# Bucket mask of an attention kernel built from per-bit rows on VectorE instead of two one-hot products on TensorE

## The reference

```
q_bits = (q @ proj > 0);  k_bits = (k @ proj > 0)        # 6 bits per row
q_bucket = sum(q_bits * 2**n);  k_bucket = sum(k_bits * 2**n)
mask = q_bucket[:, None] == k_bucket[None, :]
scores = where(mask, scale * q @ k.T, -1e9)
attn = exp(scores - max(scores));  attn = attn / (sum(attn) + 1e-9)
out = attn @ v                                            # (2, 8, 768, 64)
```

## Time and profile before

| what | value |
|---|---|
| median of three runs | 616.67 us |
| profiled execution | 616.41 us, of which the span of the trace is 614.7 us |
| attention stage in the trace | first `scores` at 13.15 us, last transposes of pair 8 near 242 us |
| TensorE busy | 605.4 us, 98% of the span |
| VectorE, ScalarE, GpSimd busy | 431.1, 347.6, 349.3 us |
| granted TensorE clock | 9 (90% or more) in all 40 slices |

### The profile page before, as it was taken

The page is one execution under the profiler, slowest core; times in us unless marked ns, Lnnn a source line. Parts: engine busy times, 40 slices in busy tenths (PEclk is TensorE's granted clock), DMA queues, the critical chain, the costliest instruction groups (busy, mean ns, idle before and its releaser), DMA issues.

```text
span 614.7 us, 10917 instructions
## 1 busy us (share of the span) xinstructions
PE 605.4 (98%) x3676; PEld 503.5 (82%) x3676; DVE 431.1 (70%) x689; ACT 347.6 (57%) x700; POOL 349.3 (57%) x337
## 2 busy tenths in 40 slices
PE   7899999999999999999999999999999999999998
PEld 3667777776776776999888999999999999988887
DVE  3988888888888885788676666545677666579920
ACT  3877777777777785354444444335444444264232
POOL 4533434333337756146458988873999999234140
PEclk9999999999999999999999999999999999999999
DMA  6842323233232210001212122113222221100202
GB/s 137 244 118 64 91 66 91 64 90 90 64 90 79 62 46 3 1 2 53 69 51 69 56 64 61 60 57 99 69 85 85 86 86 51 35 1 0 86 19 102
DMA packets 27650, 42.20 MB, mean 69 GB/s; under 512 B 3425, under 2 KB 15713, under 8 KB 27617
## 3 DMA queue, kind: packets, MB, share of 16 engines
q1 hardware_dynamic: 25648, 37.38, 20.9%
q0 software_dynamic: 1728, 4.02, 2.6%
q10 hardware_dynamic: 240, 0.39, 0.3%
HBM read 38.63 MB, written 3.15 MB: 68 GB/s over the span
## 4 chain that ended last, share of the span: by engine, by line
PE 95%; DVE 2%; DMA 1%; ACT 1%; POOL 1%; issue 0%; ACTq 0%; POOLq 0%
PE banks L1882 22%; PE banks L1914 16%; PE banks L1667 12%; PE banks L1684 11%; PE banks L1734 10%; PE banks L1996 5%; PE banks L2012 5%; PE banks L1873 4%; PE banks L1707 2%; PE banks L1818 2%; PE banks L1620 2%; DMA k_raw<-in_k 1%; PE banks L1742 1%; PE banks L1858 1%; PE banks L1626 1%; PE banks L1792 1%
## 5 line engine op out<-in xcount | busy, mean ns | idle before, releaser
L1246 DVE TENSOR_REDUCE row_min<-banks 128x1 f32<-128x768 f32 x96 | 91.8, 956 | 31.8 <-PE banks L1667 31.1
L873 ACT ACTIVATE prob<-banks,row_min 128x768 f32<-128x768 f32 x96 | 87.1, 907 | 29.0 <-DVE row_min L1246 28.9
L1506 DVE TENSOR_TENSOR partial_sums<-banks,partial_sums 128x384 f32<-128x384 f32 x78 | 43.4, 557 | 54.9 <-PE banks L1914 54.7
L1734 PE MATMUL banks<-ident,prob 128*128 128x128 f32 x576 | 79.2, 273 | 1.4 <-ACT probT L374 1.4
L1734 PEld LDWEIGHTS banks<-ident,prob 128*128 128x128 f32 x576 | 68.1, 140 | 6.7 <-issue 1.9
L606 POOL TENSOR_TENSOR k_b<-k_raw,k_a 64x768 fp32r<-64x768 f32 x16 | 29.3, 1829 | 70.7 <-ACT k_a L856 70.7
L1684 PE MATMUL banks<-probT,v_in 128*64 128x384 f32 x384 | 69.0, 494 | 0.0
L1882 PE MATMUL banks<-h_hi,w_hi 128*128 128x512 f32 (+1 forms) x256 | 66.1, 339 | 0.0
L1882 PE MATMUL banks<-h_hi,w_lo 128*128 128x512 f32 (+1 forms) x256 | 65.6, 337 | 0.0
L1882 PE MATMUL banks<-h_lo,w_hi 128*128 128x512 f32 (+1 forms) x256 | 65.3, 336 | 0.0
L374 ACT COPY probT<-banks 128x384 f32<-128x384 f32 x104 | 49.1, 480 | 22.4 <-PE banks L1734 22.1
(11 more groups left out here) (216 smaller groups left out, 1515.0 us busy)
## 6 DMA issues: line engine op xcount, KB each, us to landing
w_stage<-in_moe_w_ch SPq DMA_DIRECT2D x38, 256.0 KB, 2.6
q_raw<-in_q SPq DMA_DIRECT2D x32, 192.0 KB, 3.3
k_raw<-in_k SPq DMA_DIRECT2D x30, 192.0 KB, 3.6
w_pair<-in_moe_w_ch SPq DMA_DIRECT2D x7, 512.0 KB, 3.7
v_in<-in_v SPq DMA_DIRECT2D x16, 192.0 KB, 2.8
w_stage<-in_moe_w_ch SPq DMA_DIRECT2D x6, 512.0 KB, 3.8
out<-y_out SPq DMA_DIRECT2D x11, 256.0 KB, 2.0
seq_tables_sb<-in_dft POOLq DMA_DIRECT2D x6, 386.0 KB, 3.7
```

The costliest lines, as they stand in the source:

```text
L873: act.activation(prob[s % 2][:, :, :], s_tile(s), ACT.Exp, bias=row_min[:, s:s + 1], scale=-1.0, accum_out=row_sum[:, s:s + 1]).then_inc(e ...
L1246: dve.tensor_reduce(row_min[:, s:s + 1], s_tile(s), AX.XY, ALU.min).then_inc(min_ready, 1)
L1506: dve.tensor_tensor(out, product_bank[PRODUCT_BANK[o]], other, ALU.add).then_inc(done, 1)
L1734: op = pe.transpose(bank[:, j * P:(j + 1) * P], prob[tile % 2][:, c, j * P:(j + 1) * P], ident[:, :])
```

## The change

`bits_sb` becomes plain fp32, and the projection tables carry the six columns twice, so that B yields 12 rows of bits in each group of 32 partitions. The comparison with zero also multiplies by 1 for q and by 2^44 for k (a per-partition operand). The tasks C0 and C1 are gone from TensorE, VectorE and the bank rotation. In slots 2 and 4 VectorE runs `make_mask`: two operations on 32 partitions x 384 columns that subtract a per-partition offset, both inputs in SBUF. The q row holds bit or bit - 1, the k row -2^44 x bit or 2^44 x (1 - bit), and the product sums 2^44 times the number of bits that differ. `scores` uses 96 partitions of the second pair instead of 128.

With this sum, a row that matches no key no longer has equal scores. So VectorE runs one more small operation behind each minimum (`shift_and_scale`, 128 x 2): the minimum and -1, both times (minimum < 2^43). The exponential takes the two results as bias and as scale, where before the scale was the constant -1; it now waits for this operation.

```diff
@@ tasks and banks
-        PREPARE = {0: ["B"], 2: ["C0"], 4: ["C1"], 6: ["B"], 8: ["C0"], 10: ["C1"]}
+        PREPARE = {0: ["B"], 6: ["B"]}
         banks = [n % 3 for n in range(len(uses))]
+        if banks[-1] == banks[0]:
+            banks[-1] = banks[1]
@@ new helper
+        def make_mask(eng, h, chunk):
+            cols = slice(chunk * HALF, chunk * HALF + HALF)
+            q_rows = slice(chunk * GROUP, (chunk + 1) * GROUP)
+            k_rows = slice(D + chunk * GROUP, D + (chunk + 1) * GROUP)
+            eng.tensor_tensor(q_b[h][MASK_ROWS, cols], bits_sb[q_rows, :],
+                              bit_offset[q_rows, :].broadcast_to([GROUP, HALF]), ALU.subtract).then_inc(mask_ready, 1)
+            eng.tensor_tensor(k_b[h][MASK_ROWS, cols], bit_offset[k_rows, :].broadcast_to([GROUP, HALF]),
+                              bits_sb[k_rows, :], ALU.subtract).then_inc(mask_ready, 1)
@@ ScalarE, softmax_exp
-                need(act, min_ready, i * SLOTS + (s + 1))
+                need(act, shift_made, i * SLOTS + (s + 1))
-                act.activation(prob[s % 2][:, :, :], s_tile(s), ACT.Exp, bias=row_min[:, s:s + 1],
-                               scale=-1.0, accum_out=row_sum[:, s:s + 1]).then_inc(exp_done, 1)
+                act.activation(prob[s % 2][:, :, :], s_tile(s), ACT.Exp, bias=row_shift[:, s, 0:1],
+                               scale=row_shift[:, s, 1:2], accum_out=row_sum[:, s:s + 1]).then_inc(exp_done, 1)
@@ VectorE
-                    op = dve.tensor_scalar(bits_sb[:, :], src, 0.0, None, ALU.is_gt)
-                    dve.tensor_scalar(q_b[h][low, cols], src[top, :], code_ones[top, :], None, ALU.is_equal)
-                    op = dve.tensor_scalar(k_b[h][low, cols], src[low, :], code_ones[low, :], BIG,
-                                           ALU.not_equal, ALU.mult)
+                dve.tensor_scalar(bits_sb[:, :], scratch(i, use), 0.0, bit_size[:, :], ALU.is_gt, ALU.mult)\
+                   .then_inc(scratch_free[bank_of(i, use)], 1)
+            def shift_and_scale(i, s):
+                dve.wait_ge(min_ready, i * SLOTS + (s + 1))
+                dve.scalar_tensor_tensor(row_shift[:, s, :], row_min[:, s, 0:1].broadcast_to([P, 2]), BIG / 2,
+                                         row_min[:, s, :], ALU.is_lt, ALU.mult).then_inc(shift_made, 1)
                     if last < 2:
                         row_minimum(i, s)
+                        shift_and_scale(i, s)
+                    h, nxt = head_of(s)
+                    if s % 6 in (2, 4) and last + nxt < 2:
+                        if s % 6 == 2:
+                            wait_drained(dve, i, (s - 2, "B"))
+                        make_mask(dve, h, (s % 6) // 4)
@@ VectorE, before pair 0
-            for task in prologue:
-                prepare(-1, (0, task))
+            prepare(-1, (0, "B"))
+            dve.wait_ge(offset_loaded, 16)
+            wait_drained(dve, -1, (0, "B"))
+            for chunk in range(2):
+                make_mask(dve, 0, chunk)
@@ TensorE
-                return pe.matmul(scratch(i, use), codes[:, int(use[1][1]), :], bits_sb[:, :], start=True, stop=True)
+                    need(pe, mask_ready, 4 * (operands(i, h) + 1))
-                for lhs, rhs, start in ((q_a[h], k_a[h], True), (q_b[h], k_b[h], False)):
+                upper = slice(0, D + GROUP)
+                for lhs, rhs, start in ((q_a[h], k_a[h], True), (q_b[h][upper], k_b[h][upper], False)):
-            keep_busy(2)
-            pe.wait_ge(codes_loaded, 16)
-            prepare(-1, (0, "C0"))
-            prepare(-1, (0, "C1"))
-            for blocks in (3, 3):
+            for blocks in (3, 3, 3, 3):
                 keep_busy(blocks)
```

More of the change, by code:

```diff
@@ L43, in attention_fft_ffn_gate_kernel @@
     GROUP = 32
+    MASK_ROWS = slice(D, D + GROUP)
     NC1 = S // 2 + 2
@@ L352, in operands @@
             return i * 2 + h
-        def prepared(i, s, task):
-            if s >= 6:
-                return i, (next(x for x in range(6) if task in PREPARE.get(x, [])), task)
-            if isinstance(i, int) and i == 0:
-                return -1, (0, task)
-            return i - 1, (next(x for x in range(6, SLOTS) if task in PREPARE.get(x, [])), task)
         def drain_prob(eng, copy, i, use):
@@ L1634, in prepare @@
                 wait_free(i, use)
[L1635 to L1649 removed]
+                if isinstance(i, int) and i < 0:
+                    pe.wait_ge(top_scaled, 1)
+                else:
+                    need(pe, q_scaled, operands(i + nxt, h) + 1)
+                bits(i, use, h).then_inc(scratch_full[bank_of(i, use)], 1)
             def scores(i, s):
@@ L2086, in bucket_tables @@
     import numpy as np
-    number = np.arange(P - dim)
-    has = (number[None, :] >> np.arange(bits)[:, None]) & 1
-    codes = np.zeros((P, 2, P), np.float32)
-    for chunk in range(2):
-        codes[32 * chunk:32 * chunk + bits, chunk, :dim] = 2 * has - 1
-        codes[64 + 32 * chunk:64 + 32 * chunk + bits, chunk, dim:] = 2 * has - 1
-    ones = np.zeros((P, 1), np.float32)
-    ones[:dim, 0] = ones[dim:, 0] = has.sum(axis=0)
-    return codes, ones
+    size, offset = np.ones((P, 1), np.float32), np.zeros((P, 1), np.float32)
+    size[dim:] = 2.0 ** 44
+    for group in range(0, P, P // 4):
+        if group < dim:
+            offset[group + bits:group + 2 * bits] = 1.0
+        else:
+            offset[group:group + bits] = 2.0 ** 44
+    return size, offset
 _INS = ["q", "k", "v", "proj", "moe_w_ch1", "moe_w_ch2", "moe2_w_val", "moe2_conv_w", "moe2_w_out"]
```

76 lines of the change are left out of this document (27 added, 49 removed).

## The result

The changed kernel takes **633.89 us** (median of 4 runs, 633.45 to 634.05), the kernel before 616.79 on the same chip: a ratio of **1.0276, 95% interval 1.0258 to 1.0294**. The forecast was 631.0, in a range of 619 to 638. The profiled execution took 633.79, with a span of 631.8; that of before was 614.7, so 17.1 us are to be found.

The account below looks back on a forecast made before the run. TensorE was taken as the bound, with 95% of the chain of waits. Start 3.0, half 0 1.9, halves 1 to 14 7.7 and half 15 2.0 sum to 14.6 on 616.41, giving 631.0 us; range 619 to 638.

Parts of the forecast that it names:

- Part 1: Halves and start: 32 bucket products of 0.17 us leave TensorE, 5.4 us; C0's saved in slot 2 if nothing waits.
- Part 2 (a): Each slot: the small operation behind the minimum takes 0.19 us, lengthening the path from scores to exponential by 0.22.
- Part 2 (b): Each slot: the exponential's scale as a per-row operand adds 0.09 us, bounds 0 and 0.18.
- Part 3: Masks on VectorE: four operations per half replace four no shorter ones, hidden beside TensorE's work at no cost.
- Part 4: Slot 3: GpSimd's low part of q holds the small operation; +0.53 per half, taken as 0.55 for halves 1 to 14, 7.7 us.
- rival 1: GpSimd's instruction on 64 partitions holds nothing, parts 1 to 3 stand: 619.2 us; chance 0.13.
- 0.6 to 0.9: Sign in the timeline: duration in us of slot 3's small operation, where others last 0.19.
- a half of 14.9: Sign in the chain of waits: a half lasts 14.9 us, with ScalarE and VectorE pieces in it.
- Part 5: Start: four masks alternate with GpSimd, first scores +3.0 us; half 0 another +1.9, bounds 0.9 and 2.8.
- Part 6: Half 15: small operations held by GpSimd's nearly back-to-back instructions, +2.0 us, bounds 0.3 and 4.
- Rival 2: Loop of slots 3 to 5: the small work hides and the removed products win, 612.5 us; chance 0.05.
- Rival 3: GpSimd wins the gap: the held operation stays behind a second instruction, 1.5 us more per half, 652 us; chance 0.03.

Follow-up runs that it names:

- mask_only: Changed kernel without the small operation and with the exponential's scale constant, leaving out the uniform softmax of rows without a partner; 619.44 us.
- scale_operand: mask_only with the exponential's scale read from a row of minus ones in SBUF instead of a constant; 621.60 us.
- shift_psum: Changed kernel with the minimum and -1 in PSUM, so the small operation has one SBUF input instead of two; 627.41 us.
- filler: Changed kernel with ten filler products on TensorE before its first scores instead of four; 632.13 us.
- before_shift: Kernel before, products kept, plus the small operation (its threshold never acts) and the exponential's scale by row; 632.38 us.
- q_low_late: Changed kernel with GpSimd's low part of q made to wait for the small operation of slot 3 or 9; 639.78 us.
- clamp: Changed kernel with one VectorE pass clamping scores to 2^43 in PSUM and taking the row minimum, instead of the small operation; 620.10 us.
- clamp_offset_order: clamp_offset plus one GpSimd wait: the first batch's column folds start after the masks of slot 10 of the last full pair; 614.67 us.
- direct: Changed kernel with masks made straight from the bits in PSUM, in slots 0 and 1, without the copy of the bits; 669.36 us.
- clamp_offset: clamp with the start's four masks reading their offset from PSUM, as in offset_psum; 616.11 us.
- offset_psum: Changed kernel with the start's four masks reading their offset from PSUM; 630.06 us.
- clamp_order_filler: clamp_offset_order with six filler products at the start instead of four; 614.06 us.

## Why the prediction was right, point by point

The mechanisms stood. Several sizes were off, in both directions, and the total came out well partly because they cancel.

- **Part 1 and C0's 0.17:** with no small operation the products are worth 0.28 per half (mask_only against before). In the changed kernel slots 0 to 2 should have come down to 7.33 and take 7.40 to 7.45, so 0.10 of C0's 0.17 was not saved. "If nothing waits there", the text said; something does. In the half shown PV's piece of the chain is 2.16 with 0.02 of issue before it, where it was 2.09, behind the P1 copy that the small operation delays (see scale_operand). Part 2 had written that VectorE's next operation starts later, and put no price on it.
- **Part 2 (a), the small operation:** 0.16 long, taken at 0.19; the exponential starts 0.03 after its end. With nothing held, slots 3 to 5 were forecast to end 4.36 + 2.75 = 7.11 behind the start of slot 3; shift_psum has 7.13 to 7.16. So the loop was sized right. The sum of parts 1 and 2, forecast at +0.07, is +0.17 on average (14.58 against 14.42) for the reason above, and in the odd halves, from one of which the forecast was made, +0.29 (14.64 against 14.35).
- **Part 2 (b), the operand:** 0.09 forecast, 0.087 to 0.093 measured, and once per half. There was some luck in it: the two rows compared differ in function and in where they read as well.
- **Part 3, masks hidden:** right in steady halves, wrong where GpSimd works without a pause. There they are held (1.16 and 1.54 in half 12, 1.68 and 2.05 in half 13).
- **Part 4, the hold:** the mechanism is right, and rival 1 (none on half the partitions; the text calls it the second in one place) is out: GpSimd's instruction on 64 partitions held a VectorE operation until 0.03 past its end. This is the term that was sized wrong. In half 7 the small operation lasts 0.56 and not 0.70, since GpSimd's instruction ended 2.47 behind the start of slot 3 (129.00 - 126.53) and not 2.59 (9.92 - 7.33), and the operation wanted to start 0.02 later; in even halves it lasts 0.47 to 0.48. Slots 3 to 5 take 7.38 where 7.56 was forecast. Half 7 lost 0.46 where 0.53 was forecast. The even halves lost only 0.27, mostly because they were 0.15 longer before, which one half taken for all could not show. Together that is 3.5 us in halves 2 to 11 instead of 5.3. Of the signs named, "0.6 to 0.9" was missed, and "a half of 14.9" nearly met. The page named there, "SBUF — State Buffer" of the Trainium skill, "Who interferes with whom", was the better guide than the missing row: the trace agrees with it at 64 partitions.
- **Part 5, start and half 0:** +3.0 forecast for the first scores. Counted from GpSimd's first low part it is +3.10 (7.02 against 3.92), with the alternation mask by mask as written. That the first minimum moved by 2.90 is a sum with luck in it: the low clock adds 0.7 behind the first scores, and the low part started 0.91 earlier in this trace. Half 0: +1.9 forecast, +3.02 measured, of which 1.2 is the granted clock; filler, without that, has +1.82. In that half the small operation of slot 3 lasts 1.16, a hold of 1.0 where 0.6 to 0.7 was put. The clock had stood in the text only as something that widens the range, with at most 3 us; it cost 1.9.
- **Part 6 and the end of part 4:** halves 12 to 14 were counted as steady, at 1.6 together, and cost 5.7. In half 15 I had counted 2.0, and it cost 1.2. GpSimd's busy stretch begins in the last full pair, with the row folds, and the masks, which I had put down as hidden, meet it there. Half 1 cost 0.75 for the same 0.55.
- **Rival 2 (faster)** failed where it was said to: unheld, the small operation and the operand lengthen slots 3 to 5 from 6.77 to 7.13 or more, and C1's removal had left 0.08 to 0.19. **Rival 3** did not occur in the places I looked at in the changed kernel: in half 7, at the start and in halves 12 and 13 each held operation got in behind the GpSimd instruction that held it. As a rule it does not hold. In before_shift a held operation stayed behind two more instructions (3.48 us), in q_low_late behind one more (2.39 us). What decides between the two stays open.

Forecast 14.6 and measured 17.1 to 17.2: start and half 0 +1.0, halves 1 to 11 -1.8, halves 12 to 14 +4.1, half 15 -0.8. The total came nearer than its terms.

## What to carry to other kernels

Before a VectorE operation without a PSUM operand is added, list what GpSimd runs at the same time in *every* stretch, the first and the last too: the price is GpSimd's remaining time, not the operation's, and with GpSimd instructions back to back it can be several of them. Where two such engines meet there are three ways out: one operand in PSUM (shift_psum, 6.5 us less), a fused pass over data that is read anyway (clamp, 13.8 less), or a wait that parts them (clamp_offset_order, 1.4 less). But look at what queues behind the wait: q_low_late lost 5.9 us by it. A count over many halves should start from more than one half. And work that is freed late can stall TensorE twice, once by the wait and once by the clock behind it.

## What the runs showed of the hardware

- An operation of 128 x 2 elements, 0.16 us long, lasted up to 1.18 us beside GpSimd in the changed kernel, 2.39 in q_low_late and 3.48 in before_shift, where it was held over two and three GpSimd instructions; with one operand in PSUM it took 0.22 everywhere. The same held for masks on 32 partitions at the start: 1.43 to 2.06 us, against 0.55 with the offset in PSUM, beside the same GpSimd instructions. GpSimd's own instructions became longer in exchange: 1.94 and 2.00 instead of 1.82.
- VectorE's pass that clamps and reduces 768 columns in PSUM in place takes 962 ns, against 952 for the reduction alone, plus 133 ns for reading the result.
- A second operand per row costs the exponential 0.09 us (907 to 1000 ns).
- In the profiled executions the granted clock fell to its lower level behind pauses of TensorE of 4.32 us (after), 2.30 (direct, where the PV piece that followed took 3.70 us), 2.14 (clamp_offset_order) and 1.78 (before_shift). It stayed at 1.00 behind pauses of 1.50 (clamp_offset), 1.21 (filler) and 1.17 (offset_psum), and with no pause (clamp_order_filler). The Trainium skill, page "TensorE: Matmul & The Clock Gate", "What's actually happening", has an idle array fall back to half clock, and the rows of the falls agree.
